# Attention in half-sequence tasks of one head pair, with score and value products on 64-wide parts of the array

## Time and profile before

| | us |
|---|---|
| median of three runs | 849.26 |
| lowest and highest | 848.99, 853.97 |
| span of the profiled execution | 853.1 |
| TensorE busy in it | 785.4 |
| attention alone, up to the first product of the first mixture | 0 to 88.7 |
| attention with groups 0 and 1 | 88.7 to about 184 |

### The profile page before, as it was taken

One profiled execution on the slowest core, in us unless ns is written; L12 is line 12 of the kernel. 1 busy time (PEld: TensorE's weight loads), 2 busy tenths in 40 slices (PEclk: granted clock), 3 DMA queues, 4 the chain that ended last, 5 costly groups with the idle time before them and its releaser, 6 DMA issues.

```text
span 853.1 us, 12740 instructions
## 1 busy us (share of the span) xinstructions
PE 785.4 (92%) x4197; PEld 701.5 (82%) x4198; DVE 351.8 (41%) x793; ACT 290.4 (34%) x606; POOL 84.3 (10%) x131
## 2 busy tenths in 40 slices
PE   5686999999999999999999999999999469899995
PEld 4575888989989989889899899898998357677774
DVE  4667555522234212144112143222225529853961
ACT  4867554511123001023011032021112237734751
POOL 3111000000000000000000000001010214322431
PEclk9878999999999999999999999999999679999998
DMA  9565331020022000022000022112022259860920
GB/s 225 158 147 141 76 75 29 24 99 1 1 99 99 0 1 0 0 98 74 25 0 0 0 70 79 60 65 75 1 75 99 74 188 319 307 224 21 327 87 16
DMA packets 75121, 73.73 MB, mean 86 GB/s; under 512 B 50724, under 2 KB 53028, under 8 KB 75088
## 3 DMA queue, kind: packets, MB, share of 16 engines
q1 hardware_dynamic: 72784, 71.03, 26.4%
q0 software_dynamic: 2304, 2.27, 0.8%
HBM read 68.04 MB, written 9.29 MB: 91 GB/s over the span
## 4 chain that ended last, share of the span: by engine, by line
PE 78%; DMA 6%; DVE 6%; issue 4%; ACT 4%; POOL 1%; POOLq 1%; SPq 0%; DVEq 0%; ACTq 0%
PE ps L963 23%; PE ps L965 23%; PE ps L964 23%; DMA out_rows<-acc,id_scatter 4%; DMA acc<-x_rows,id_gather 2%; PE ps L1016 2%; PE ps L996 2%; ACT acc L481 1%; PE ps L1123 1%; PE ps L982 1%; DVE w_lo L734 1%; PE ps L1006 1%; DVE w_lo L738 1%; DVE xt_lo L696 1%; PE ps L1113 1%
## 5 line engine op out<-in xcount | busy, mean ns | idle before, releaser
L540 ACT ACTIVATE h_hi<-ps 128x384 fp32r<-128x384 f32 x128 | 63.0, 492 | 384.7 <-PE ps L965 384.7
L963 PE MATMUL ps<-w_hi,h_hi 128*128 128x512 f32 x472 | 186.6, 395 | 1.3 <-issue 1.3
L965 PE MATMUL ps<-w_hi,h_lo 128*128 128x512 f32 x472 | 184.6, 391 | 0.0
L964 PE MATMUL ps<-w_lo,h_hi 128*128 128x512 f32 x472 | 184.4, 391 | 0.0
L963 PE MATMUL ps<-xt_hi,w_hi 128*128 128x384 f32 (+1 forms) x512 | 174.0, 340 | 0.0
L965 PE MATMUL ps<-xt_hi,w_lo 128*128 128x384 f32 (+1 forms) x512 | 171.8, 336 | 0.0
L964 PE MATMUL ps<-xt_lo,w_hi 128*128 128x384 f32 (+1 forms) x512 | 171.6, 335 | 0.0
L743 DVE SCALAR_TENSOR_TENSOR h_lo<-ps,h_hi 128x384 fp32r<-128x384 f32 x128 | 71.3, 557 | 178.3 <-ACT h_hi L540 178.2
L963 PEld LDWEIGHTS ps<-w_hi,h_hi 128*128 128x128 f32 x472 | 89.1, 189 | 20.4 <-issue 3.0
L965 PEld LDWEIGHTS ps<-w_hi,h_lo 128*128 128x128 f32 x472 | 88.9, 188 | 19.0
L964 PEld LDWEIGHTS ps<-w_lo,h_hi 128*128 128x128 f32 x472 | 88.9, 188 | 17.6
(11 more groups left out here) (147 smaller groups left out, 801.1 us busy)
## 6 DMA issues: line engine op xcount, KB each, us to landing
stage<-in_moe_w SPq DMA_DIRECT2D x60, 512.0 KB, 4.7
acc<-in_moe_w SPq DMA_DIRECT2D x36, 512.0 KB, 6.4
stage<-in_k SPq DMA_DIRECT2D x16, 192.0 KB, 3.1
stage<-in_q SPq DMA_DIRECT2D x16, 192.0 KB, 3.4
stage<-in_v SPq DMA_DIRECT2D x8, 384.0 KB, 4.4
x_rows<-acc SPq DMA_DIRECT2D x4, 768.0 KB, 3.6
out_rows<-acc SPq DMA_DIRECT2D x4, 768.0 KB, 5.2
acc<-in_v SPq DMA_DIRECT2D x32, 72.0 KB, 2.2
```

The costliest lines, as they stand in the source:

```text
L540: nc.scalar.activation(h_hi[:, f, :], ps[:, f % 2, 0:GT], ACT.Relu).then_inc(h_hi_ok, 1)
L963: mm(dst, a_hi, b_hi, start=start, stop=False)
L964: mm(dst, a_hi, b_lo, start=False, stop=False)
L965: return mm(dst, a_lo, b_hi, start=False, stop=stop)
```

## The change

Attention becomes 16 tasks in place of 8 iterations. A task is one batch element, one half of the sequence and one pair of heads; the order is all four pairs of the first half, then all four pairs of the second half, then the same for batch element 1. Keys are transposed once for a pair (in the tasks of a first half) and kept for both halves (`k_low`, `k_high`); queries are transposed three pieces a task. `q_diag` is gone: the scores come from 12 products a task of 64 dimensions x 64 queries by 120 keys, one for each unit and head, which go in turn to the four 64 x 64 parts of the array. A row group of the softmax is now one head and two units, and there are six a task as before there were six in half an iteration. The value products are 12 a task, 120 rows x 64 dimensions by 64 queries, in turn on the two 64-column halves of the array.

The products with `mean_mat` are gone. The block means of v are made on GpSimd by five additions that halve a row of 32 x 64 numbers and one scaling, for four heads at a time (96 partitions), and two DMAs a task bring them under the windows of v. GpSimd also makes the high parts of expert 0's weights, which ACT made before.

Tasks 0 to 3 hold attention alone. Tasks 4 to 15 run with groups 0, 1 and 2 of expert 0, one group in four tasks, with four and three steps a task in turn. Group c waits until the outputs of tasks 4c to 4c+3 are split. Group 3 and the rest follow.

```diff
+    PARTS = 2
+    PS = S // PARTS
+    UH = UNITS // PARTS
+    UP = UH // 2
+    TH = PS // P
+    PREPS = B * PAIRS
+    TASKS = PREPS * PARTS
+    LEAD = PAIRS
...
+    def task(a):
+        return a // (PARTS * PAIRS), a // PAIRS % PARTS, a % PAIRS
...
+    def wide(a):
+        return a < LEAD
...
+                                         ap=[[DH, WK], [UQ * DH, count], [1, DH]])).then_inc(win_in[a % 2], 16)
+            def load_sums(a):
+                b, s, n = task(a)
+                c = b * PAIRS // 2 + n // 2
+                sp.wait_ge(vsum_ok, c + 1)
+                for h in range(2):
+                    row = NB * (2 * (n % 2) + h)
+                    sp.dma_start(v_all[a % 2][WK:KW, :, h * DH:(h + 1) * DH],
+                                 v_sum[row:row + NB, c:c + 1, :].broadcast_to((NB, UH, DH))).then_inc(win_in[a % 2], 16)
...
+            first_w1(3)
+            load_queries(5)
+            load_windows(4)
+            load_sums(4)
+            first_w2(0)
+            first_w2(1)
             sp.dma_start(dp[:, :, :], dprobs.rearrange("(t p) e -> p t e", p=P)).then_inc(dp_in, 16)
+            load_values(2)
+            first_w2(2)
+            load_queries(6)
+            load_windows(5)
+            load_sums(5)
+            first_w2(3)
...
+            for a in range(7, TASKS):
+                b, s, n = task(a)
+                if b and s == 0 and n:
+                    load_keys(prep(a))
+                load_queries(a)
+                load_windows(a - 1)
+                load_sums(a - 1)
+            load_windows(TASKS - 1)
...
+            def sum_values(c):
+                gp.wait_ge(v_in, 16 * c + 16)
+                left = BLOCK * DH
+                for j in range(STEPS - 1):
+                    left //= 2
+                    if j or c:
+                        gp.wait_ge(vsum_step, STEPS * c + j)
+                    nc.gpsimd.tensor_tensor(v_rows[0:VR, 0:left], v_rows[0:VR, 0:left], v_rows[0:VR, left:2 * left], ALU.add).then_inc(vsum_step, 1)
+                gp.wait_ge(vsum_step, STEPS * c + STEPS - 1)
+                nc.gpsimd.tensor_scalar(v_sum[0:VR, c, :], v_rows[0:VR, 0:DH], 1.0 / BLOCK, None, ALU.mult).then_inc(vsum_step, 1)
+                gp.wait_ge(vsum_step, STEPS * c + STEPS)
+                gp.sem_inc(vsum_ok, 1)
+            def high_w1(c):
+                gp.wait_ge(w1_in[c], 16)
+                nc.gpsimd.tensor_copy(w1_hi[:, c, :], early_w1(c)).then_inc(w1_hi_ok, 1)
+            def high_w2(c):
+                gp.wait_ge(w2_in[c], 16)
+                nc.gpsimd.tensor_copy(w2_hi[:, 2 * c:2 * c + 2, :].rearrange("p j d -> p (j d)"), early_w2(c)).then_inc(w2_hi_ok, 1)
+            sum_values(0)
+            high_w1(0)
+            sum_values(1)
+            for c in range(1, PIECES):
+                high_w1(c)
+            high_w2(0)
+            high_w2(1)
+            sum_values(2)
+            high_w2(2)
+            high_w2(3)
...
+            def copy_keys(a):
+                m, n = prep(a), task(a)[2]
+                act.wait_ge(tk_done, m + 1)
+                if a:
+                    act.wait_ge(scores, 2 * a)
+                at = bank_k(a) * 512
+                def windows(t0, count):
+                    src = ps_flat[:, at + win(t0):at + win(t0) + WK]
+                    return bass.AP(tensor=src.tensor, offset=src.offset, ap=[list(src.ap[0]), [UQ, count], [1, WK]])
+                nc.scalar.activation(k_low[:, 0, 0:WK], ps_flat[:, at:at + WK], ACT.Copy)
+                nc.scalar.activation(k_low[:, 1:UH, 0:WK], windows(1, UH - 1), ACT.Copy)
+                nc.scalar.activation(k_high[n][:, 0:UH - 1, 0:WK], windows(UH, UH - 1), ACT.Copy).then_inc(k_copied, 1)
...
+            def high_o(a):
+                b, s, n = task(a)
+                act.wait_ge(pv_done, a + 1)
+                nc.scalar.activation(xt_hi[:, b * PAIRS + n, s * PS:(s + 1) * PS], ps[:, 7, 0:PS], ACT.Copy).then_inc(o_hi, 1)
+            def attend(a, fill):
+                if a:
+                    high_o(a - 1)
+                if a + 1 < TASKS:
+                    if task(a + 1)[1] == 0:
+                        copy_keys(a + 1)
+                    copy_queries(a + 1)
+                exps(a, 1)
+                fill(0)
+                evac_t(a, 0)
+                if a + 1 < TASKS:
+                    exps(a + 1, 0)
+                fill(1)
+                evac_t(a, 1)
+                fill(2)
+                fill(3)
...
+            def low_o(a):
+                b, s, n = task(a)
+                dve.wait_ge(o_hi, a + 1)
+                cols = (slice(None), b * PAIRS + n, slice(s * PS, (s + 1) * PS))
+                TT(xt_lo[cols], ps[:, 7, 0:PS], xt_hi[cols].bitcast(F32), ALU.subtract).then_inc(o_lo, 1)
+            def attend(a, fill):
+                more = a + 1 < TASKS
+                if a:
+                    low_o(a - 1)
+                if more and task(a + 1)[1] == 0:
+                    keys(a + 1)
+                if wide(a):
+                    mask(a + 1, 0)
+                    norm(a, 1)
+                    mask(a + 1, 1)
+                    norm(a + 1, 0)
+                    return
+                norm(a, 1)
+                fill(0)
...
+            mask(0, 0)
+            mask(0, 1)
+            norm(0, 0)
+            for a in range(LEAD):
+                attend(a, lambda j: None)
+                low_w1(0, early_w1, [a])
             dve.wait_ge(dp_in, 16)
...
+            def qk(a):
+                pe.wait_ge(q_copied, a + 1)
+                pe.wait_ge(k_ok, prep(a) + 1)
+                if a:
+                    pe.wait_ge(masked, 2 * UP * a)
+                for u in range(UH):
+                    for h in range(2):
+                        rows, half = slice(h * DH, (h + 1) * DH), slice(u % 2 * UQ, (u % 2 + 1) * UQ)
+                        last = mm(ps[half, bank_s(h), u // 2 * KW:(u // 2 + 1) * KW], q_t[rows, u * UQ:(u + 1) * UQ], keys_of(a)[rows, u, :],
+                                  start=True, stop=True)
+                        if u == UH - 1:
+                            last.then_inc(scores, 1)
+            def turn(a, h):
...
+            def pv(a):
+                pe.wait_ge(pt_ready, 2 * a + 2)
+                pe.wait_ge(win_in[a % 2], 16 * 5 * (a // 2 + 1))
+                if a:
+                    pe.wait_ge(o_lo, a)
+                for u in range(UH):
+                    for h in range(2):
+                        last = mm(ps[h * DH:(h + 1) * DH, 7, u * UQ:(u + 1) * UQ], v_all[a % 2][0:KW, u, h * DH:(h + 1) * DH],
+                                  pr_t[h][0:KW, u * UQ:(u + 1) * UQ], start=True, stop=True)
                 last.then_inc(pv_done, 1)
...
+            def attend(a, fill):
+                more = a + 1 < TASKS
                 if more:
+                    if task(a + 1)[1] == 0:
+                        transpose_keys(a + 1)
+                    transpose_queries(a + 1)
+                fill(0)
+                turn(a, 0)
                 if more:
+                    qk(a + 1)
+                fill(1)
+                turn(a, 1)
+                fill(2)
+                pv(a)
+                fill(3)
+            def periods(q):
+                return [(a, 4 - (a % 2)) for a in range(LEAD + PAIRS * q, LEAD + PAIRS * (q + 1))]
...
                 pe.wait_ge(w1_ok, PIECES * e + PIECES)
+                if first:
+                    pe.wait_ge(o_lo, PAIRS * (c + 1))
...
+            pe.wait_ge(s_ident, 2)
+            transpose_keys(0)
+            transpose_queries(0)
+            qk(0)
+            for a in range(LEAD):
+                attend(a, lambda j: None)
+            for c in range(G - 1):
+                step = group_steps(c, 0, c // HALVES, c % HALVES, True)
+                for a, most in periods(c):
+                    attend(a, lambda j: next(step, None) if j < most else None)
+            for _ in group_steps(G - 1, 0, B - 1, HALVES - 1, True):
                 pass
```

More of the change, by code:

```diff
@@ new lines, in copy_queries, with exps @@
+            def copy_queries(a):
+                act.wait_ge(tq_done, a + 1)
+                if a:
+                    act.wait_ge(scores, 2 * a)
+                nc.scalar.activation(q_t, ps[:, bank_q(a), 0:PS], ACT.Copy, scale=-SCALE).then_inc(q_copied, 1)
+            def exps(a, h):
+                for j in range(UP):
+                    act.wait_ge(masked, 2 * UP * a + UP * h + j + 1)
+                    p = pr[a % 2][:, UP * h + j, :]
+                    nc.scalar.activation(p, p, ACT.Exp, bias=nmax[:, a % 2, h, j:j + 1], scale=-1.0, accum_out=rsum[:, h, j:j + 1]).then_inc(exped, 1)
@@ L576, in slots1 @@
                 return stage[:, c, :]
-            for c in range(HALVES, G):
-                group(c, 0, False)
+            group(G - 1, 0, False)
             split_w1(1, slots1)
@@ L808, in group @@
                     add_rows(c, e, g, tt, fresh)
-            for g in range(HALVES, G):
```

(33 more changed lines are left out.)

546 lines of the change are left out of this document (192 added, 354 removed).

## The result

The changed kernel takes **828.83 us**, the median of four runs (827.96 to 832.16); the kernel before took 849.12 (848.42 to 853.97) beside it. The ratio is 0.976, with an interval of 0.972 to 0.979: faster by 20.3 us, where the prediction had 840 and a gain of 9.3. The direction and the range held; the size of the gain is twice what the sum gave. The profiled execution spans 826.1 us against 853.1.

What follows compares the result with a forecast made beforehand. An engine-to-engine chain bounds attention alone, TensorE's work the stage among mixture steps. Alone 55 us for 88.7 (minus 33.7), among steps plus 24.2, net minus 9.5: median 849.3 becomes 840 us, range 817 to 860.

Steps and rivals of the forecast that it cites:

- What bounds the kernel: Whole kernel: an engine-to-engine chain bounds attention alone up to 88.7 us; TensorE's work bounds the stage among mixture steps.
- the pitch of the narrow products: Score and value runs among mixture steps: 0.055 us a record, 1.32 a run of 24, 30.4 us for 23 runs.
- The lower bound of 0.027: Score and value records: 0.027 us each if four parts of the array work fully side by side.
- The change of shape: TensorE going in and out of narrow runs among mixture steps: 0.31 us a pair, 7.1 us for 23 runs.
- Waits and a slow start: Attention among mixture steps: 3 us for task outputs, 1.6 for keys, 1 for a slow clock at the start.
- Attention alone: First stage: a chain of 10.5 us a task with half the time slow; first mixture product at 55 us, not 88.7.
- Means on GpSimd at no cost: Block means on GpSimd: 2.4 to 9.6 us a set of four heads, estimated 4.4, ready before the first value run.
- The clock: Sign against the forecast: TensorE's first stage at full clock throughout would give back 6 us.
- Side by side: Rival: all four array parts load and multiply together, 0.027 us a record, run 0.65; 820 us, chance 0.24.
- No overlap: Rival: narrow products on different parts do not overlap, score records 0.10 us, run 2.4; 857 us, chance 0.17.
- in turn: Rival: each weight load waits for the product before it, 0.15 us a score record, 0.11 a value record; 895 us, chance 0.05.
- The start bound by loads: Rival: loads or GpSimd bound the first stage, first mixture product at 65 us; 850 us, chance 0.12.

Runs made afterwards that it cites:

- experiment 1: Changed kernel with the load of `dp` moved earlier, behind the queries of task 1; 822.53 us, ratio 0.967 to the kernel before.
- experiments 9 and 10: Changed kernel with the earlier `dp` load, plus 15 (9) or 9 (10) unread products a task in tasks 0 to 3; 825.18 and 821.73 us.
- experiment 2: Changed kernel with score and value products reordered so that neighbours use the same part of the array; 844.85 us, ratio 0.992 to the kernel before.
- 5 to 7: Changed kernel with only score products reordered: heads in turn, units in turn within a head, another rotation of four parts; 830.95, 830.06 and 828.53 us.
- Experiment 12: Changed kernel with score products on two diagonal parts in turn, neighbours writing one PSUM bank, output not the reference's; 830.81 us.
- experiment 4: Kernel before with only its score and value products made narrow, on diagonal parts, and TensorE's loop over iterations 1 to 3 written out; 851.4 us, ratio 1.000.

## Why the prediction was wrong in size

**What bounds the kernel: right.** The split into a stage bound by a chain and one bound by TensorE held, and with it the form of the sum: time up to the first mixture product, plus TensorE's attention work behind it.

**The step that failed is the pitch of the narrow products: "the load of 128 weight columns sets the pitch", and from it "I take 0.055 for both kinds: products overlap, loads queue".** Measured are 0.0325 us for a score record and 0.035 for a value record: loads overlap too. The row it was taken from the earlier trace rows shows products that load 128 columns over 128 rows each, the whole array, so it cannot tell whether loads to other parts queue; the experiments on order show that they do not at 0.055. The lower bound of 0.027 was the better one. The terms: 11 score runs at 0.78 for 1.32 give 5.9 us, 12 value runs at 0.85 for 1.32 give 5.6.

**The change of shape** was 7.1 us from 0.31 a pair; it is 0.20 beside a run, 2.5 us less. The mean products of the earlier trace rows took 0.10 more than their number of records at 0.11, which the narrow runs need not pay. That it costs at all was right. The sum is not even here: what it charges behind a narrow run it leaves out behind the three mean runs of the kernel before, 0.6 us in all.

**Waits and a slow start** were 5.6 us; all pauses of TensorE after the first mixture product come to 2.0 up to 230 us, and the slow clock costs 2.7 (up to 63.8 us, 12 mixture products take 4.2 us for 2.1, three transposes 0.64 for 0.33 and the score run 1.11 for 0.78). That is 4.7, so this term gives the last 0.9: 5.9 + 5.6 + 2.5 + 0.9 = 14.9, the difference between 24.2 and 9.3. With the 0.6 above it is 15.5, so the account closes to 0.6 us.

**Attention alone: 57.85 for 55.** The chain of a task came out right within 1 us, in part by luck: half of the time was counted at the slow clock, the rows show it nearly throughout, and against this the runs were shorter than counted, 1.48 at half clock, where 1.3 had been taken for full clock and twice that for half. `dp`, of which the prediction says "At 50 us it is just in time", came at 56.2: the sum counts the bytes ahead of it, and nothing for the 6.1 us in which SP issues the loads ahead of it. DVE waited 4.9 us, and experiment 1, without that wait, starts the mixture 3.8 us sooner; the sum had 2.2 for `dp` and the low weights together.

**Means on GpSimd at no cost: right for TensorE, which never waits for them, but not in price, and not for DVE.** An addition of 1024 columns takes 2.36 us, so a set of four heads about 6, within the bounds of 2.4 and 9.6. The Trainium skill (GPSIMD Engine Reference, 3.1 Elementwise) has 4497 ns for 2048 float32; the trace agrees.

Two lines of the changed kernel show what the prediction has nothing for:

```profile
24.66 5.42 POOL L445 TENSOR_TENSOR acc<-acc 96x1024 f32<-96x1024 f32 x5 [7.76 <-DMA acc<-in_v]
...
25.78 1.31 DVE L722 COPY k_low<-k_sum 128x144 f32<-128x144 f32 x1
```

The same copy takes 0.22 us at 15.38 and 0.23 at 37.32. It stands in the chain of keys, and the scores behind it come 11.5 us after those before, not 10.5. That GpSimd's additions hold it is read from the timeline.

**The clock.** "if TensorE's first stage ran at full clock throughout, which would give back 6" is not refuted by experiments 9 and 10, though they gain nothing: their added products stand in the chain for about that much. From score to score, tasks 1 to 4 take 26.0 us in experiment 9, 23.7 without the 2.3 behind added products, for 30.3 in experiment 1, of which 1.4 are a slower DVE copy; about 5 us is an estimate, from these numbers, of what the full clock is worth over these three. No run has the clock without the products.

**The rivals.** *Side by side* had 0.24 and 820 us; it came nearest in mechanism, with 0.78 us for the 0.65 that it asked of a run. *No overlap* and *in turn* are excluded for four parts by experiments 2 and 5 to 7: the price of no overlap is 0.064, not 0.10, so even that rival would have ended at about 845 and not at 857. *The start bound by loads* was a small part of the truth, by one late 48-column load and not by bytes. The Trainium skill (TensorE: Matmul & The Clock Gate, Part 3) speaks of many products running at the same time in the array; this case's runs agree in kind, with a factor of 2.0 for four parts (1.54 over 0.78) and 1.5 for two, short of four and two.

## What to carry to other kernels

When products use a part of the array, put neighbours on different parts, and take the pitch of a run from start to start before counting on it; for the scores, four parts in turn gave twice the speed of one, for an edit in the order of a loop. A row of wide products does not price narrow ones, neither in stream nor in load: keep the full range between "side by side" and "one after another" until a run of narrow products has been measured. Here the value lay near the lower end, and only for one of the orders tried. A small load that an engine waits for in the middle of its program holds all that stands behind it; look for the first use of each load, and count the time in which the queue issues the loads ahead of it, not only their bytes. Products that only hold the clock belong where nothing waits behind them. When the column of the clock and the durations of one and the same run disagree, go by the durations.

## What was not expected of the hardware

- A float32 record of 120 columns on a 64 x 64 part takes 0.064 us at full clock when the same part is used over and over (experiment 2; 2.81 us for 24 at half clock, 0.117 each), where one on the whole array takes 0.11.
- Two parts in turn overlap by 1.5, in rows, in columns or on the diagonal, in one bank or in two (1.03 us for a run of 24 scores each time, where the same part takes 1.54; the value run, on column halves, has 0.85 for 1.36). The Trainium skill (TensorEngine Tiling (Array Packing), Gotcha 1: PSUM Pressure) says that different row tiles can't reach the same PSUM bank at one time. Experiment 12 had neighbours of different rows in one bank and shows no cost of it; experiment 4, also in one bank, was slow for a reason that is not known.
- With GpSimd at work, some of DVE's operations on 3 to 48 columns went from about 0.2 us to between 0.7 and 1.1 (0.78, 0.72 and 1.00 in experiment 9, 1.13 in 10), and one of 360 columns in the changed kernel from 0.53 to 2.56, by its timeline:

```profile
77.93 5.59 POOL L445 TENSOR_TENSOR acc<-acc 96x1024 f32<-96x1024 f32 x3 [4.58 <-DMA acc<-in_v]
77.94 0.18 DVE L741 RECIPROCAL rinv<-rsum 128x3 f32<-128x3 f32 x1
78.15 2.56 DVE L743 TENSOR_TENSOR h_rows<-h_rows,rinv 128x360 f32<-128x360 f32 x1
```

  The reciprocal beside it keeps its 0.18. The Trainium skill (SBUF — State Buffer, SBUF: two separate sides) names a port pair that GpSimd shares with DVE operations on two SBUF inputs and those in a two-port mode, held for a whole instruction; the traces agree as to which operations are slowed. No run takes GpSimd's work away, so this is a reading.
